# Moving the preparation of the next block, the turning of x and the waits of the output groups in a fused attention and expert kernel

## The reference

```python
for t in range(S):
    kt, vt, bt = (k_n[:, :, t], v[:, :, t], beta[:, :, t, None])
    y[:, :, t] = np.einsum('bhd,bhde->bhe', q[:, :, t], state)
    v_old = np.einsum('bhde,bhd->bhe', state, kt)
    state = state + bt[:, :, :, None] * np.einsum('bhd,bhe->bhde', kt, vt - v_old)
...
gate = 1.0 / (1.0 + np.exp(-(x @ w_gate)))
val = x @ w_val
return (gate * val @ w_out)
...
e_idx = np.argmax(logits, axis=1)
...
h = np.maximum(xc[mask] @ w1[e], 0.0)
y[mask] = gate_w[mask, None] * (h @ w2[e])
out[do_compute] = xc + y
```

## Time and profile before

| | us |
|---|---|
| median of 3 runs | 972.34 (971.52 to 973.3) |
| profiled execution | 972.34 |
| its span, first to last instruction | 970.5 |
| TensorE busy | 937.8 |
| VectorE busy | 451.0 |
| mean granted TensorE clock | 0.982 |

### The profile page before, as it was taken

How to read it: one execution, slowest core, us unless ns; L and a number is a source line. 1 busy time by engine, 2 the same in 40 slices (tenths; PEclk the granted TensorE clock), 3 DMA queues, 4 the chain that set the end, 5 groups by cost and what they waited for, 6 DMA issues and landing times.

```text
span 970.5 us, 23070 instructions
## 1 busy us (share of the span) xinstructions
PE 937.8 (97%) x10087; PEld 628.4 (65%) x10087; DVE 451.0 (46%) x1100; ACT 163.5 (17%) x346; POOL 105.3 (11%) x136
## 2 busy tenths in 40 slices
PE   4999999999999999999999999999999999999995
PEld 4965665666566566666666665666555688778874
DVE  7967654765657366836752773222012211211121
ACT  2221211221131121122112211211111121111110
POOL 2010010011010001101010101001001222222221
PEclk7799999999999999999999999999999999999998
DMA  8830022005000400230041000001900115551400
GB/s 351 326 116 1 27 78 88 26 3 148 17 27 15 151 26 1 91 100 2 2 148 42 1 2 34 18 1 28 394 19 9 53 48 204 204 192 43 153 26 28
DMA packets 30299, 78.75 MB, mean 81 GB/s; under 512 B 4072, under 2 KB 20120, under 8 KB 29312
## 3 DMA queue, kind: packets, MB, share of 16 engines
q1 hardware_dynamic: 20112, 61.46, 17.9%
q10 hardware_dynamic: 6912, 9.55, 2.7%
q0 software_dynamic: 3184, 6.39, 2.2%
HBM read 65.34 MB, written 13.00 MB: 81 GB/s over the span
## 4 chain that ended last, share of the span: by engine, by line
PE 91%; DVE 4%; DMA 2%; POOL 1%; issue 1%; SPq 0%; ACT 0%; DVEq 0%; POOLq 0%
PE ps L1102 20%; PE ps L1089 19%; PE ps L1078 18%; PE ps L1156 10%; PE ps L1168 9%; PE ps L987 2%; PE ps L945 2%; PE ps L1043 2%; DMA prod<-in_turned_moe_w_out 1%; PE ps L1002 1%; PE ps L959 1%; PE ps L971 1%; PE ps L1017 1%; PE ps L1032 1%; PE ps L1049 1%; POOL length L405 1%
## 5 line engine op out<-in xcount | busy, mean ns | idle before, releaser
L1078 PE MATMUL ps<-xT,shared 128*128 128x384 f32 x576 | 204.0, 490 | 0.7 <-ACT xT L864 0.7
L1089 PE MATMUL ps<-xT,shared 128*128 128x384 f32 x576 | 204.5, 491 | 0.1
L1102 PE MATMUL ps<-wo,prod 128*128 128x393 f32 x576 | 202.4, 501 | 0.0
L697 DVE TENSOR_TENSOR prod<-sig,ps 128x384 f32<-128x384 f32 x96 | 52.9, 552 | 235.2 <-PE ps L1089 234.5
L1078 PEld LDWEIGHTS ps<-xT,shared 128*128 128x128 f32 x576 | 107.4, 190 | 72.4 <-issue 1.0
L1089 PEld LDWEIGHTS ps<-xT,shared 128*128 128x128 f32 x576 | 107.1, 190 | 70.8 <-issue 0.4
L1102 PEld LDWEIGHTS ps<-wo,prod 128*128 128x128 f32 x576 | 105.7, 189 | 71.5 <-issue 0.6
L1156 PEld LDWEIGHTS ps<-xgT,arena 128*128 128x128 f32 x816 | 95.3, 195 | 5.1 <-ACT xgT L892 0.8
L1156 PE MATMUL ps<-xgT,arena 128*128 128x128 f32 x816 | 95.6, 278 | 0.6 <-ACT xgT L892 0.6
L869 ACT ACTIVATE sig<-ps 128x384 f32<-128x384 f32 x96 | 47.2, 491 | 278.8 <-PE ps L1078 278.8
L1168 PE MATMUL ps<-arena,hT 128*128 128x384 f32 x272 | 90.5, 486 | 0.0
(11 more groups left out here) (171 smaller groups left out, 693.1 us busy)
## 6 DMA issues: line engine op xcount, KB each, us to landing
arena<-in_moe_w SPq DMA_DIRECT2D x16, 1536.0 KB, 10.4
arena<-in_kq SPq DMA_DIRECT2D x7, 1536.0 KB, 7.5
x_scratch<-x ACTq DMA_DIRECT2D x24, 196.5 KB, 3.6
arena<-in_kn SPq DMA_DIRECT2D x8, 576.0 KB, 3.9
shared<-in_v SPq DMA_DIRECT2D x8, 576.0 KB, 7.0
arena<-in_kr SPq DMA_DIRECT2D x8, 576.0 KB, 5.4
out<-x ACTq DMA_DIRECT2D x24, 192.0 KB, 2.5
prod<-in_turned_moe_w_out SPq DMA_DIRECT2D x1, 2304.0 KB, 13.1
```

The source lines that it names most:

```text
L697: nc.vector.tensor_tensor(prod[:, f, :], sig[:, f % 2, :], ps_m[3 - f % 2][:, 0:CT], ALU.mult)\
L1078: last = nc.tensor.matmul(ps_m[f % 2][:, 0:CT], wg[:, a, f * P:(f + 1) * P], xT[:, a, :], start=(a == 0), stop=(a == KT - 1))
L1089: last = nc.tensor.matmul(ps_m[3 - f % 2][:, 0:CT], wv[:, a, f * P:(f + 1) * P], xT[:, a, :], start=(a == 0), stop=(a == KT - 1))
L1102: last = nc.tensor.matmul(ps_m[t][:, 0:XW], prod[:, a, t * P:(t + 1) * P], wo[:, a, :], start=(a == 0), stop=(a == NF - 1))
```

## The change

It moves work in five places and leaves all arithmetic as it is.

- In a round, off 1 follows off 0 after one or two dense groups, norm and the first two grams stand together behind a further group, and the third gram one group later. Before, a gram stood directly behind each off block, and norm behind the third gram. The banks of the grams and their waits follow from it. The scan begins a group or two earlier, so its steps fall between other groups.
- x_turn becomes three pieces, one for each third of `xT`, each with its own copy by ScalarE. For blocks 1 to 7 they share the bank `ps_m[3]` and stand behind parts 0, 1 and 2 of the last output tile. For block 0 they are side by side in three banks. The first gate group waits for all three copies.
- The first output group of a round waits until all twelve products are made. Before, each part of the first tile waited for its own three.
- SP loads kq behind kr, once the last write of the earlier block is done, instead of ahead of it, once the last read is.
- The first gather waits for the saved rows ahead of GpSimd's copy of the indices instead of behind it.

```diff
--- before.py
+++ after.py
@@ -48,8 +48,8 @@
                 pieces.append(("rank", q - 1, 0))
             if q == Q - 1:
                 pieces += [(stage, q, 0) for stage in early.get((t, part), ())]
-            if t == TT - 1 and part == 1 and q + 1 < Q:
-                pieces.append(("x_turn", q + 1, 0))
+            if t == TT - 1 and part < 3 and q + 1 < Q:
+                pieces.append(("x_turn", q + 1, part))
     return pieces
 
 
@@ -104,7 +104,7 @@
         if step != scan(0)[-1]:
             order.append(("warm", 1, 1))
         behind(0.3)
-    order += [("x_turn", 0, 0)] + [("pt", 1, i) for i in range(3)]
+    order += [("x_turn", 0, a) for a in range(KT)] + [("pt", 1, i) for i in range(3)]
     for c in range(Q):
         q = c + 1
         pieces = dense_pieces(c, Q, NF, TT)
@@ -117,18 +117,15 @@
             order.append(("from_lanes", q, 0))
             dense(3.0 if late else 2.0)
             order.append(("off", q, 0))
+            dense(1.2)
+            order.append(("off", q, 1))
+            dense(1.1)
             if follows:
-                order += [("gram", q + 1, 0), ("pt", q + 1, 0)]
-                dense(2.0)
-                order += [("off", q, 1), ("gram", q + 1, 1), ("pt", q + 1, 1)]
-                dense(2.0)
-                order += [("gram", q + 1, 2), ("norm", q + 1, 0), ("pt", q + 1, 2)]
+                order += [("norm", q + 1, 0), ("gram", q + 1, 0), ("gram", q + 1, 1), ("pt", q + 1, 0)]
                 dense(1.0)
+                order += [("gram", q + 1, 2), ("pt", q + 1, 1), ("pt", q + 1, 2)]
+                dense(0.7)
                 later = prepare(q + 1)
-            else:
-                dense(1.2)
-                order.append(("off", q, 1))
-                dense(1.1)
             steps = scan(q)
             gap = max(0.7, (sum(p[0] not in light for p in pieces) - 4.0) / len(steps))
             for step in steps:
@@ -359,7 +356,7 @@
 
     def gram_banks(q, i):
 
-        first = (0, 2, 4 if q == 0 else 0)[i] if q < 2 else (2, 0, 0)[i]
+        first = 4 if (q, i) == (0, 2) else 2 * (i % 2)
         return ps[:, first:first + 2]
 
     def quarters(t):
@@ -463,13 +460,12 @@
         def gather(t):
             nc.gpsimd.tensor_copy(idx_g[:], ids[:, bass.ds(t, 1)]).then_inc(idx_ready, 1)
             copied()
-            if isinstance(t, int) and t == 0:
-                for part in range(TT):
-                    pool.wait_ge(x2_saved[part], 16 * Q)
             nc.gpsimd.indirect_dma_start(
                 xg[:, :], None, x2_d[:, :], bass.IndirectOffsetOnAxis(ap=idx_g[:, 0:1], axis=0),
                 bounds_check=last_free, oob_is_err=False).then_inc(x_in, 16)
 
+        for t in range(TT):
+            pool.wait_ge(x2_saved[t], 16 * Q)
         gather(0)
         pool.wait_ge(x_turned, 1)
         pool.wait_ge(x_kept, 1)
@@ -535,10 +531,9 @@
         load_kn(1)
         for q in range(2, Q):
 
-            sp.wait_ge(q_done, reads(JS * (q - 1) - 1))
-            load_kq(q)
             sp.wait_ge(y_done, JS * (q - 1))
             load_kr(q)
+            load_kq(q)
             load_v(q)
             sp.wait_ge(dt_ready, q)
             load_kn(q)
@@ -679,7 +674,7 @@
                     nc.vector.tensor_tensor(y, y, own_y, ALU.add).then_inc(y_copied, 1)
                 else:
                     if s:
-                        dve.wait_ge(xt_done, s // JS)
+                        dve.wait_ge(xt_done, KT * (s // JS))
                     dve.wait_ge(y_done, s + 1)
                     nc.vector.tensor_copy(y, own_y).then_inc(y_copied, 1)
 
@@ -849,7 +844,7 @@
             elif stage == "read":
                 s = q
                 if i == 0:
-                    act.wait_ge(xt_done, s // JS)
+                    act.wait_ge(xt_done, KT * (s // JS))
                 elif s < JS:
                     act.wait_ge(filled, 32)
                 act.wait_ge(q_done, reads(s))
@@ -859,9 +854,9 @@
 
         def mlp(stage, q, f):
             if stage == "x_turn":
-                act.wait_ge(xt_done, q + 1)
-                for a in range(KT):
-                    nc.scalar.activation(xT[:, a, :], ps_a[:, a, 0:CT], ACT.Copy).then_inc(xt_copied, 1)
+                bank = ps_m[3] if q else ps_m[f]
+                act.wait_ge(xt_done, KT * q + f + 1)
+                nc.scalar.activation(xT[:, f, :], bank[:, 0:CT], ACT.Copy).then_inc(xt_copied, 1)
             elif stage == "gate":
                 act.wait_ge(gate_done, NF * q + f + 1)
                 if NF * q + f >= 2:
@@ -928,10 +923,10 @@
                     pe.wait_ge(kq_first[i], 16)
                 elif i == 0:
                     pe.wait_ge(kq_in[q % 2], 16 * ((q + 1) // 2))
-                if q >= 2 and i == 1:
-                    pe.wait_ge(y1_ready, q)
-                elif q >= 2 and i == 2:
-                    pe.wait_ge(pt_ready, 3 * q + 2)
+                if q >= 2 and i < 2:
+                    pe.wait_ge((y1_ready, tt_ready)[i], q)
+                elif q >= 2:
+                    pe.wait_ge(pt_ready, 3 * q + 1)
                 elif q == 1:
                     pe.wait_ge(raw_copied, (3, 3, 4)[i])
                 banks = gram_banks(q, i)
@@ -963,7 +958,7 @@
                 pe.wait_ge(y1_ready, q + 1)
                 pe.wait_ge(dt_ready, q + 1)
                 if q:
-                    pe.wait_ge(pt_ready, min(3 * q + 4, 3 * Q))
+                    pe.wait_ge(y_copied, JS * q)
                 for m in range(CN):
                     for g in range(G2):
                         for h in range(HH):
@@ -1048,19 +1043,26 @@
                 for _ in range(f):
                     nc.tensor.matmul(ps_m[3][:, 0:2 * P], ident[:], wo_t[:, 0, 0:2 * P], start=True, stop=True)
             elif stage == "x_turn":
-                if q == 0:
-                    pe.wait_ge(ident_ready, 1)
-                    pe.wait_ge(router_copied, 1)
-                pe.wait_ge(y_copied, JS * (q + 1))
-                pe.wait_ge(st_ready, writes(JS * (q + 1) - 1))
+                bank = ps_m[3] if q else ps_m[f]
+                if f == 0:
+                    if q == 0:
+                        pe.wait_ge(ident_ready, 1)
+                    pe.wait_ge(y_copied, JS * (q + 1))
+                    if q == 0:
+                        pe.wait_ge(router_copied, 1)
+                    if q >= 2:
+                        pe.wait_ge(rank_read, q - 1)
+                elif q:
+                    pe.wait_ge(xt_copied, KT * q + f)
                 for j in range(JU):
                     t = slice(j * C, (j + 1) * C)
-                    nc.tensor.transpose(ps_a[:, 0, t], yo[0:C, j, 0:P], ident[0:C, 0:C])
-                    nc.tensor.transpose(ps_a[:, 2, t], yo[C:P, j, CG * W2 - P:CG * W2], ident[C:P, C:P])
-                for j in range(JU):
-                    t = slice(j * C, (j + 1) * C)
-                    nc.tensor.matmul(ps_a[0:C, 1, t], yo[0:C, j, P:CG * W2], ident[0:C, 0:C], start=True, stop=True)
-                    last = nc.tensor.matmul(ps_a[C:P, 1, t], yo[C:P, j, 0:C], ident[C:P, C:P], start=True, stop=True)
+                    if f == 0:
+                        last = nc.tensor.transpose(bank[:, t], yo[0:C, j, 0:P], ident[0:C, 0:C])
+                    elif f == 2:
+                        last = nc.tensor.transpose(bank[:, t], yo[C:P, j, CG * W2 - P:CG * W2], ident[C:P, C:P])
+                    else:
+                        nc.tensor.matmul(bank[0:C, t], yo[0:C, j, P:CG * W2], ident[0:C, 0:C], start=True, stop=True)
+                        last = nc.tensor.matmul(bank[C:P, t], yo[C:P, j, 0:C], ident[C:P, C:P], start=True, stop=True)
                 last.then_inc(xt_done, 1)
             elif stage == "gate":
                 if f == 0:
@@ -1068,21 +1070,18 @@
                         pe.wait_ge(w_in, 32)
                     else:
                         pe.wait_ge(x2_copied, TT * (q - 1) + 1)
+                    pe.wait_ge(xt_copied, KT * (q + 1))
                 elif f == 1 and q:
                     pe.wait_ge(x2_copied, TT * (q - 1) + 2)
                 elif f >= 2:
                     pe.wait_ge(sig_ready, NF * q + f - 1)
                 for a in range(KT):
-                    if f == 0:
-                        pe.wait_ge(xt_copied, KT * q + a + 1)
                     last = nc.tensor.matmul(ps_m[f % 2][:, 0:CT], wg[:, a, f * P:(f + 1) * P], xT[:, a, :],
                                             start=(a == 0), stop=(a == KT - 1))
                 last.then_inc(gate_done, 1)
             elif stage == "val":
                 if f >= 2:
                     pe.wait_ge(prod_ready, NF * q + f - 1)
-                elif f == 0 and q >= 2:
-                    pe.wait_ge(rank_read, q - 1)
                 elif f == 1 and q:
                     pe.wait_ge(x2_copied, TT * q)
                 for a in range(KT):
@@ -1091,13 +1090,11 @@
                 last.then_inc(val_done, 1)
             elif stage == "out":
                 t, part = f
```

(11 more changed lines are left out.)

## The result

| | before | after |
|---|---|---|
| median in us | 972.82 (971.52 to 974.24, 4 runs) | 981.13 (978.68 to 982.84, 4 runs) |
| profiled execution | 972.34 | 981.73 |
| its span | 970.5 | 979.7 |

The changed kernel takes 1.0087 times as long, with an interval of 1.0068 to 1.0104: some 8.5 us more. The forecast was 981.4 us. It was made on one execution, the profiled one of before, and that of after is 9.4 us longer, with 9.2 us between the two spans. These 9.2 are made of three stretches, read from the starts of TensorE's records: the start, up to the first gate group, +2.5; the eight rounds, up to the first expert matmul, +8.34; the expert layer -1.6.

A forecast was written before the change was run, and what follows sets the result against it. TensorE, busy for 97% of the span, was taken as the bound, so added instructions and waits in its queue are paid in full. Terms 5.6 + 0.2 + 1.3 - 3.5 - 1.2 + 0.3 + 0.0 + 5.9 + 0.5 = +9.1 on 972.34: 981.4 us, range 976.5 to 987.5.

The forecast's parts named there:

- turning of x: Rounds 0 to 6: lost pairing and two more blocks cost 0.80 us a time, +5.6 us.
- first turning: Before round 0: loses the pairing, 0.4 us, but its copies begin sooner, +0.2 us.
- preparation, with round 0: Next block's preparation: added blocks +1.3, masked scores -3.5, transposes -1.2 and +0.3; round 0's write and freed wait cancel.
- wait for all products: First output group of a round: 0.95 us in each of rounds 2 to 7, 0.2 in round 1, +5.9 us.
- gather: At the end: the index copy now waits for the saved rows, adding 0.2 to 0.95, taken as +0.5 us.
- Rival 1: Cheap pieces: six transposes on one half take 0.26 us, switches 0.10, gather 0.2; about 977.5 us; chance 0.14.
- block's price: TensorE: each block interrupting dense work costs 0.19 us, 0.09 before it and 0.10 in the group behind.
- Rival 2: Third gram waits behind norm (+3.0), or each block pays a 0.12 us handover (2.5 for 21); 984 to 987; chance 0.13.
- Rival 3: Last product ready before TensorE reaches the output group, so the 5.9 us falls away: 975.5 us; chance 0.05.
- masked scores: Read of a step: the last masking ends about 0.9 us before the read needs it, giving back 3.5 us.
- the transposes: Block 3's first stage: round 3 no longer waits for lane transposes, -1.2 us; round 2 waits about 0.3 instead.
- third gram's margin: Third gram's wait for the first masking is hidden with 0.24 us to spare, costed at nothing.

The follow-up runs named there:

- e2: Kernel before with only the turning of x split into three pieces, each with its own copy: 979.31 us beside 976.5, ratio 1.0043.
- e8: Kernel before with the turning of x still one block, but its transposes no longer paired across array halves: 977.27 us beside 972.75, ratio 1.0052.
- e10: Kernel before with only the new preparation order, its banks and waits; repeat of e4: 966.84 us beside 972.75, ratio 0.9939.
- e7: Kernel before with the new preparation and the wait for all twelve products, x turned in one block: 973.64 us beside 973.23, ratio 1.0002.
- e1: Changed kernel with the output and rank groups' waits as before, so no wait for all products: 980.53 us beside 976.5, ratio 1.0041.
- e3: Kernel before with only the first output group's wait changed, to all twelve products: 976.78 us beside 976.5, ratio 1.0009.
- e5: Kernel before with only GpSimd's waits for the saved rows moved ahead of its copy of the indices: 973.04 us, ratio 1.0006.
- e4: Kernel before with only the new preparation order, its banks and waits; same kernel as e10: 969.79 us beside 976.5, ratio 0.9933.

## Why the prediction was right, step by step

The mechanism is right: a full queue on TensorE, to which the change adds blocks and waits. Most of the terms are near. That the total is off by only 0.6 us is in part luck: turning, first turning and wait came out 1.2 us dearer than forecast, and the preparation gave back 1.8 us more.

| term | forecast | measured | from |
|---|---|---|---|
| turning of x, 7 times | +5.6 | +6.2 | 0.88 each: rows of after, e2, e8 |
| first turning | +0.2 | +0.3 | last write's start to first gate group's, 3.74 to 4.06; means +0.2, see below |
| preparation, with round 0 | -3.1 | -4.9 | e10 |
| wait for all products | +5.9 | +6.4 | e7 against e10, without the gather's 0.2; e1 gives 6.3 without round 1 |
| gather | +0.5 | +0.5 | this pair, 3.03 to 3.51; means of three and ten traces +0.3 |
| sum | +9.1 | +8.5 | beside it, after against before: rounds +8.3, first turning +0.3 |

**The turning.** The choice of 0.47 for six unpaired transposes lay between 0.42 and 0.52; they take 0.51 and 0.52. In these runs each half of the array keeps its own pace, which was the upper bound of the two near ones. Rival 1 (0.26) falls with this. Its 977.5 was also worked out wrongly: a switch at 0.10 was set in for the seven blocks of the preparation alone. For all 21 it would be 981.4 - 2.9 - 1.9 - 0.3 = 976.3, just below the range. The block's price came as read from the earlier trace rows: 423.58 to 425.76 is 2.18, where two output groups without a block stand 1.99 apart. Rival 2's handover of 0.12 more a block is not there: e2 less e8 is 0.35 to 0.45 a round for two blocks, 0.39 in the mean. The Trainium skill, "TensorEngine Tiling (Array Packing)", Key Properties, says that a change of tiling mode drains the engine; the traces agree that a block has a price, 0.19 us for the way in and out, but none shows a drain as its cause. The estimate of 0.33 from the Trainium skill, "TensorE: Matmul & The Clock Gate", Single matmul latency, was too much.

**The first turning.** In the traces with pieces (after, e1, e2) it takes 4.06 us from the last write's start to the first gate group; in the nine traces with the old one block there it takes 3.74 to 4.00, 3.86 in the mean. So its own price is nearer to 0.2, as forecast.

**The wait for all products.** Its path was right: the last matmul's result, VectorE's product of 0.55, TensorE's start 0.05 later. The distance from val to output grew by 0.88 to 0.89 in five rounds. The group behind the wait is slow like one behind a block (493.83 to 495.93 is 2.10, in e1 492.04 to 494.02 is 1.98), for which 0.07 was taken without a row; together 0.98 to 0.99 a round rather than 0.95. One round went otherwise than "VectorE isn't behind there" had it. In round 3 the last product started at 401.84, although val's result was out at 401.35. A solve step of two times 0.32 ended at 400.24, and behind it VectorE had sat idle for 1.60, so it was not solve work that held it. What held it isn't named by the trace: the product needs val's last record too, and the row blames that. It cost 0.38 once, in after and in e7 alike, and its cause stays open. Rival 3, the product in time, is out by e3 and e7.

**The preparation** was worth 1.8 us more than forecast, and this is the largest miss. The masked scores (-3.5, four waits) and the transposes (1.2 to 0.2, forecast 0.3) came as worked out, and the third gram's margin of 0.24 came out as 0.26. Three things were left out or mis-sized:

- The grams. Their cost was priced for the cover ("two grams (2.16)") but not put into the sum. Three single grams take 3 x 1.14 = 3.42, a pair and a single 2.08 + 1.14 = 3.22: 0.20 less in each of six rounds, -1.2. The 0.19 for an interruption was counted at every added block, and what the joining of two grams saves was not set against it.
- A wait costs more than its bracket. In round 4 of before the gate group at 444.32 was followed by the read at 447.43 (row below), 3.11 later; after, 448.02 to 450.15 is 2.13. That is 0.98 for a bracket of 0.90, since the bracket begins only at the modelled end of the group. Over four waits it is 0.3.

```profile
447.43 1.15 PE L987 MATMUL ps<-st,arena 48*64 48x48 f32 x64 [0.90 <-DVE arena L617]
```

- Round 0. The forecast was +0.7 for the write that waits for ScalarE and -0.7 for the wait given back. The write waits 1.40, since ScalarE copies an output tile and issues its two DMAs ahead of the copy. The timeline of ScalarE in after:

```profile
134.29 0.50 ACT L872 ACTIVATE x<-ps 128x393 f32<-128x393 f32 x1 [1.66 <-PE ps L1099]
134.82 0.36 ACTq L875 DMA_DIRECT2D x_scratch<-x  x1
135.21 0.46 ACTq L876 DMA_DIRECT2D out<-x  x1
135.72 0.49 ACT L843 ACTIVATE ub<-ps 128x384 f32<-128x384 f32 x1 [0.93 <-PE ps L997]
```

The apply was done at 134.87, the copy began at 135.72. Here, from before round 0 where ScalarE had nothing else in its queue, were the wrong neighbour: 0.7 more. Against it a wait of 0.28 for `shared` went, too.

By these, -3.1 - 1.2 - 0.3 + 0.4 = -4.2 of the measured -4.9 are named. Some 0.3 of the rest lies in before's round 1, which took 89.64 in e5's trace and 89.90 in this one. The last 0.4 has the size of three small things that TensorE's starts show. In round 1 of before a val group takes 2.33 us, 0.2 more than such a group elsewhere, as the read behind it waits for the state; in e10 it doesn't. The wait for the transposes went from 1.27 to 0.27 by the starts, 0.1 more than the forecast -0.9. And one gate group in round 4 of before takes 2.16 where 2.04 is usual.

**The gather** could not be settled by its time. This pair of traces shows 0.5; the means leave 0.3, of which a part may be chance.

**Times and rounds.** The times of e4 and e10 fell by 6.0 to 6.5 us, the rounds by 4.9. The times of e8 rose by 5.1 (3.3 to 6.8), its rounds with the last part by 3.6. Those of e2 rose by 4.2, its rounds by 6.2. Each difference is near the size of the stretches of the next section, and it isn't shown that they are its cause.

## What to carry to other kernels

When an order of work is changed, list what stands between each producer and each consumer before and after: a wait that costs nothing where a block covers it (e3) costs 1 us a round once the new order takes the cover away (e7). Put the savings of joined blocks into the sum with the same care as the prices of added ones, and read a price from a neighbour whose other engines have the same queue. And split a change before it is judged: its preparation alone is 0.6% faster than the kernel before; its turning and its wait for all products are what make the whole slower.
